# Sums of weights and low parts of keys and queries on GpSimd instead of VectorE

## The reference

```python
p_packed = sm_attn(p, k, v)              # 8 batches, 8 heads, 576 keys, head size 64
x = sm_attn(q, p_packed, p_packed)
h = x @ w_in                             # 512 -> 2048
y = (max(h, 0) + alpha * min(h, 0)) @ w_out
g = y @ w_gate                           # 512 -> 1536
out = (g * sigmoid(g) * (y @ w_val)) @ w_down
```

## Time and profile before

| | |
|---|---|
| three runs, us | 1558.52, 1558.85, 1555.52; median 1558.52 |
| profiled execution, us | 1558.1 |
| its span (first to last instruction), us | 1556.3 |
| TensorE busy, us | 1548.7 |
| VectorE busy, us | 1110.5 |
| ScalarE busy, us | 708.1 |
| GpSimd busy, us | 176.7 |
| granted clock of TensorE over the span | 1.000 |

### The profile page before, as it was taken

The page is one execution under the profiler, slowest core; times in us unless marked ns, Lnnn a source line. Parts: engine busy times, 40 slices in busy tenths (PEclk is TensorE's granted clock), DMA queues, the critical chain, the costliest instruction groups (busy, mean ns, idle before and its releaser), DMA issues.

```text
span 1556.3 us, 24850 instructions
## 1 busy us (share of the span) xinstructions
PE 1548.7 (100%) x9328; PEld 1435.6 (92%) x9328; DVE 1110.5 (71%) x1956; ACT 708.1 (45%) x1427; POOL 176.7 (11%) x194
## 2 busy tenths in 40 slices
PE   9999999999999999999999999999999999999999
PEld 6999999999999999999988888888888889999999
DVE  5565669877988779888755686557765685677666
ACT  4565567555765567655522252124422251234223
POOL 2654341000000010023200000000000000000000
PEclk9999999999999999999999999999999999999999
DMA  7443323442544345358466666676676668877866
GB/s 269 131 131 120 91 85 113 137 129 87 166 130 136 113 165 169 102 198 296 161 238 226 217 210 194 228 255 204 176 243 224 216 203 261 306 266 247 285 232 195
DMA packets 134503, 294.07 MB, mean 189 GB/s; under 512 B 13472, under 2 KB 44208, under 8 KB 134384
## 3 DMA queue, kind: packets, MB, share of 16 engines
q1 hardware_dynamic: 122400, 249.74, 49.7%
q0 software_dynamic: 11840, 42.48, 7.1%
q10 hardware_dynamic: 144, 0.26, 0.0%
HBM read 240.53 MB, written 51.90 MB: 188 GB/s over the span
## 4 chain that ended last, share of the span: by engine, by line
PE 96%; DVE 3%; DMA 1%; ACT 0%; issue 0%; DVEq 0%; ACTq 0%
PE acc L1070 14%; PE h L846 10%; PE h L848 10%; PE h L847 10%; PE side L846 9%; PE side L847 9%; PE side L848 9%; PE acc L1074 7%; PE acc L846 5%; PE acc L848 5%; PE acc L847 5%; DVE mixed L1536 1%; PE side L1004 1%; DVE piece L1536 1%; PE side L941 0%; DMA wring<-d_scratch 0%
## 5 line engine op out<-in xcount | busy, mean ns | idle before, releaser
L1070 PE MATMUL acc<-g,w 128*128 128x288 f32 x1792 | 272.8, 294 | 0.0
L1070 PEld LDWEIGHTS acc<-g,w 128*128 128x128 f32 x1792 | 248.9, 188 | 0.0
L1419 ACT ACTIVATE rows_b<-side 128x512 f32<-128x512 f32 (+1 forms) x60 | 33.4, 556 | 285.6 <-PE side L848 285.6
L1211 ACT ACTIVATE g<-floats 128x288 fp32r<-128x288 f32 x192 | 85.4, 445 | 165.0 <-DVE floats L1760 118.3
L1074 PE MATMUL acc<-g,w 128*128 128x288 f32 x896 | 156.2, 296 | 0.0
L846 PE MATMUL h<-attn,mixed 128*128 128x288 f32 x512 | 155.4, 303 | 0.5 <-DVE g L1536 0.5
L848 PE MATMUL h<-attn,mixed 128*128 128x288 f32 x512 | 151.1, 295 | 0.0
L847 PE MATMUL h<-attn,mixed 128*128 128x288 f32 x512 | 151.0, 295 | 0.0
L1074 PEld LDWEIGHTS acc<-g,w 128*128 128x128 f32 x896 | 131.2, 188 | 0.0
L1211 ACT ACTIVATE piece<-floats 128x512 fp32r<-128x512 f32 (+2 forms) x217 | 128.5, 616 | 3.2 <-PE side L848 2.9
L1536 DVE TENSOR_TENSOR g<-floats,g 128x288 fp32r<-128x288 f32 x192 | 87.3, 455 | 48.3 <-ACT g L1211 47.0
(11 more groups left out here) (324 smaller groups left out, 3934.8 us busy)
## 6 DMA issues: line engine op xcount, KB each, us to landing
ring<-w_scratch SPq DMA_DIRECT2D x90, 512.0 KB, 4.4
wring<-d_scratch SPq DMA_DIRECT2D x157, 256.0 KB, 2.9
ring_c<-w_scratch SPq DMA_DIRECT2D x60, 512.0 KB, 4.1
w_scratch<-piece POOLq DMA_DIRECT2D x36, 512.0 KB, 3.9
floats<-w_in SPq DMA_DIRECT2D x64, 256.0 KB, 3.1
ring_b<-w_scratch SPq DMA_DIRECT2D x30, 512.0 KB, 4.9
ring<-d_scratch SPq DMA_DIRECT2D x46, 256.0 KB, 2.9
d_scratch<-piece POOLq DMA_DIRECT2D x42, 256.0 KB, 3.5
```

The source lines that it names most:

```text
L1070: pe.matmul(acc[:, m, 0:CH], w2[:, j, x, m * P:(m + 1) * P], g[:, s % 2, 0, :], start=False, stop=False)
L1211: return nc.scalar.activation(dst, src, ACT.Copy, **kw)
```

## The change

It does three things. The four sums of each of the 18 sets are made by GpSimd instead of VectorE, in the same four operations and at the same place of the plan. The low parts of all k and q pieces are GpSimd's, so 36 pieces behind slot 63 (q of batch 3, k and q of batches 4 to 7) move; v, w, g and s pieces behind slot 63 stay with VectorE. And since sums and low parts are now on two engines, two waits change: SP, before it loads over the raw buffer of a gate tile, waits for that set's sums as well as for its low part; and the sums wait for all transposes of the first softmax before them in the plan (`turned`), as they write over its buffer, and no longer for those of the batches whose `packedT` is past. `firsts_before` goes.

```diff
 POOL_SLOTS = 64
-BY_POOL = [p for p in PIECES if p[0] in "kvqwo" and PLACE["split", p] < PLACE["y", POOL_SLOTS - 1]]
+BY_POOL = [p for p in PIECES if p[0] in "kq" or p[0] in "vwo" and PLACE["split", p] < PLACE["y", POOL_SLOTS - 1]]
...
             def load(p):
                 if RAW_NO[p] >= RING:
-                    once.wait_ge(*low_of(RAWS[RAW_NO[p] - RING]))
+                    last = RAWS[RAW_NO[p] - RING]
+                    once.wait_ge(*low_of(last))
+                    if last[0] == "g":
+                        once.wait_ge(sums_step, 4 * last[1] + 4)
...
+            def sums(e):
+
+                _, j, half = e
+                g_no, v_no = ("g", j, 0), ("g", j, 1)
...
+                if half == 0:
+                    if j in STAGED:
+                        once.wait_ge(y_stored, 16 * before(e, "ycopy"))
+                    else:
+                        once.wait_ge(turned, before(e, "turn"))
+                    if j >= EARLY_KEEPS:
+                        once.wait_ge(packed_done, B - 1)
+                    if j:
+                        once.wait_ge(*low_of(("s", j - 1, 1)))
+                    for p in (g_no, v_no):
+                        once.wait_ge(raw_landed[raw_slot(p)], landed(p))
+                    nc.gpsimd.tensor_tensor(s1_, a21, a22, ALU.add).then_inc(sums_step, 1)
+                    nc.gpsimd.tensor_tensor(s3_, a11, a21, ALU.subtract).then_inc(sums_step, 1)
+                    return
+                once.wait_ge(sums_step, 4 * j + 1)
+                nc.gpsimd.tensor_tensor(s2_, s1_, a11, ALU.subtract).then_inc(sums_step, 1)
+                once.wait_ge(sums_step, 4 * j + 3)
+                nc.gpsimd.tensor_tensor(s4_, a12, s2_, ALU.subtract).then_inc(sums_step, 1)
...
             for e in PLAN:
                 if e[0] == "split" and e[1] in BY_POOL:
                     input_low(e[1])
+                elif e[0] == "sums":
+                    sums(e)
...
-            def sums(e):
...
-                        once.wait_ge(turned, ST * firsts_before(e))
...
-                    nc.vector.tensor_tensor(s1_, a21, a22, ALU.add).then_inc(sums_step, 1)
-                    nc.vector.tensor_tensor(s3_, a11, a21, ALU.subtract).then_inc(sums_step, 1)
...
-                elif e[0] == "sums":
-                    sums(e)
```

More of the change, by code:

```diff
@@ L612, in unsplit @@
             return weight_sums(p[1])[:, 512 * p[2]:512 * p[2] + 512] if p[0] == "s" else raw(p)
-        def firsts_before(e):
-            return before(e, "packedT")
         def y_block(name, k, h):
@@ L806, in input_low @@
                                         ).then_inc(input_split, 1)
+            def sums(e):
+                _, j, half = e
+                g_no, v_no = ("g", j, 0), ("g", j, 1)
+                a11, a22 = raw(g_no)[:, 0:256], raw(v_no)[:, 256:512]
+                a12, a21 = raw(g_no)[:, 256:512], raw(v_no)[:, 0:256]
+                if j >= NT2:
+                    a12, a21 = a21, a12
+                s1_, s2_, s3_, s4_ = [weight_sums(j)[:, 256 * i:256 * i + 256] for i in range(4)]
+                if half == 0:
[16 more added lines that the diff above has]
+                nc.gpsimd.tensor_tensor(s4_, a12, s2_, ALU.subtract).then_inc(sums_step, 1)
             pool.dma_start(alphas, alpha).then_inc(alpha_landed, 16)
```

## The result

| | kernel before | changed kernel |
|---|---|---|
| median, us | 1557.12 | 1561.23 |
| lowest to highest, us | 1555.52 to 1558.85 | 1558.48 to 1563.72 |
| runs | 10 | 10 |
| span of the profiled execution, us | 1556.3 | 1559.4 |

The ratio is 1.0026, interval [1.0016, 1.0036]: 4.1 us slower, where I had forecast 0.7 us faster and no measurable change. The granted clock is 1.00 in both traces.

A forecast was written before the change was run, and what follows sets the result against it. TensorE was taken as the bound, busy 1548.7 of 1556.3 us, with VectorE seldom ending its waits. -1.6 + 0.9 = -0.7 us gave 1557.4 on the profiled execution's 1558.1, or 1557.8 as median; range 1555.4 to 1564.1 us.

The forecast's parts named there:

- (e): VectorE operations with two SBUF inputs blocked by GpSimd, at slots 84 to 86 and 64 slots later: +0.9 us.
- (a): 57 us of low parts and sums leave VectorE, relieving dense windows 400 to 440 and 600 to 640 us: -1.6 us.
- three quiet windows: Stretches from 240 us on outside the two dense windows, where TensorE was said to be never idle.
- (b): Work added to GpSimd: 36 pieces, 52.4 us, and 72 sums at 0.7 us, 50 us; it has room.
- (c): GpSimd's moved pieces and sums arrive in time; tightest piece has 3.19 us, 1.6 us left: hidden.
- (d): GpSimd's queue behind stores, and SP's extra wait before reloading a gate tile's raw buffer, cost nothing.
- a second kind of duration of the low part of g: Sign of a right forecast: some VectorE low parts of g last 0.8 to 1.4 us, which is the port.
- port rival: GpSimd takes the port ahead of needed low parts in eight stretches with k pairs: +5.6, 1564.1 us; chance 0.20.
- GpSimd late: A GpSimd piece or sum stands behind a waiting store, stalling TensorE at four tightest pieces: +4, 1562.5 us; chance 0.04.
- 0.39 us records instead of 0.47: Sign of a right forecast: TensorE's matmuls at the pieces in the dense windows shorten from 0.47 to 0.39 us.

The follow-up runs named there:

- e3: Changed kernel with each GpSimd sum waiting for the one ahead to finish, leaving a gap between any two; 1556.15 us, ratio 0.9991 to the kernel before.
- e7: Changed kernel with only one gap more, between the second and third sum, two sums staying back to back; 1557.91 us, ratio 1.0003 to the kernel before.
- e10: e3 with the low parts of the v pieces behind slot 63 moved to GpSimd as well; 1557.90 us, ratio 1.0001 to the kernel before.
- e4: Changed kernel with the float g left in PSUM up to slot 247; 1561.88 us, ratio 1.0029 to the kernel before.
- e2: Kernel before with only the k and q pieces moved to GpSimd, sums staying on VectorE; 1558.59 us, ratio 1.0007 to the kernel before.
- e1: Changed kernel with the k and q pieces back on VectorE, only the sums on GpSimd; 1561.71 us, ratio 1.0034 to the kernel before.
- e6: e3 with the k and q pieces back on VectorE, so only sums with gaps on GpSimd; 1557.82 us, ratio 1.0004 to the kernel before.
- e9: e8 with each sum also made in two halves of 128 columns with waits between; 1557.24 us, ratio 0.9999 to the kernel before.
- e8: e3 with each k and q piece behind slot 63 in two halves of 288 columns, a wait between; 1555.43 us, ratio 0.9991 to the kernel before.

## Why the prediction was wrong

**The step that failed** is (e), in its last sentence: "Elsewhere the low part of g comes 1 to 5 us early and a block of at most 1.4 us mostly vanishes in it." A block is not at most 1.4 us. I had taken the one GpSimd subtraction of the earlier trace rows for the unit of blocking. The four sums are three without a pause and one behind it, and VectorE is sure to get in only at the pause: the low part of g takes 2.16 us at slot 119, 3.23 at the longest. e3 and e7 show this, for they change nothing but the pauses. With it falls the value taken in (a): a block of 2.2 us at the sums of slots 119 and 183 is carried through a chain without slack, and -1.6 us became 2 x 0.80 = +1.6.

By the steps:

- *(a) removed, -1.6 us.* Right in kind, too large. Without the long holds (e3) the dense windows are 0.36 and 0.32 us shorter; with them 0.80 and 0.82 longer. I had costed the 57 us as leaving VectorE; 41 of them came back as waiting inside its instructions. I had also called TensorE never idle in the three quiet windows. In the kernel before, the h tile of slot 209 is 0.29 us late by its starts (665.02); in e3 it is not, and the stage from slot 192 on is 0.32 us shorter.
- *(b) added to GpSimd.* Right: 56 pieces of 576 columns, total 292 us against 280. A sum takes 0.73 to 0.74 us undisturbed, forecast 0.65 to 0.75; the means of 803 to 1116 ns are sums that VectorE held up in turn.
- *(c) in time, (d) waits and queues.* Right: no wait of TensorE on a GpSimd piece or sum shows, nor on the reload of a raw buffer. e10 shows what lies beyond.
- *(e) the port.* The mechanism was right, and what would show it also (a second kind of duration of the low part of g). The place was wrong: slots 84 to 86, where I had put 0.45 us, lie in the stage that stayed 168.87 us. The bad order did occur there. GpSimd's pieces held up a low part of g (1.69 us) and the normalisation (1.56 us for 0.75), and the next low part of g, kept out by a sum, ended at 300.35. TensorE wanted it at 300.60, so 0.25 us of the 0.54 were left, as VectorE no longer has 1.42 us of pieces to make in between. The same holds 64 slots later, and the 0.36 us of that stage lie elsewhere, at two h tiles of slots 169 and 171. The Trainium skill, "SBUF — State Buffer", section "Who interferes with whom", which I had weighed, speaks of one instruction keeping the port for its length; the row at 396.33 shows a VectorE instruction kept out for three of GpSimd's. It had waited since before the second and the third of them began, and this is so at 14 of 20 ends of a sum. The measurement goes further than the page. e4 confirms its condition, two inputs in SBUF, for this subtraction (450 ns against 604).
- *(e), size.* +0.9 us was forecast; the blocking cost 1.6 in the dense windows (and took their gain), 0.4 between them, 1.3 behind slot 192.

Of the rivals, the *port rival* was nearest (chance 0.20, 1564.1 us): slower by 4.1 us and for its reason, but it put the cost at eight pairs of k pieces. e2 shows those at +1.7 us by the table, 1.2 of it at slot 209 alone, and 1.0007 in time; the sums without a pause carry the rest (e3). Its condition, a block longer than slack plus what VectorE has saved, was the right test, and I applied it to the wrong instructions. *GpSimd late* didn't happen. The statement that the dense windows would show 0.39 us records instead of 0.47 was wrong, and this was the sign I had named. A row for the test was at hand: `sums` in the diff issues s1, s3 and s2 without a wait that can hold between them, and 3 x 0.7 us behind slot 118, ahead of a window in which VectorE has 38.96 of 40 us, needed only to be written down.

That the parts do not add up (e1 +4.8, e2 +1.7, both together +3.3) is in the main slots 85, 149 and 209, as shown at e6. What stays open: what decides whether VectorE gets in between two sums without a pause, and the single late tiles of e9 and e10. I hold the latter for places where the order of arrival at the port happens to be bad, but this is argued and not shown. GpSimd work of the same kind added without moving any wasn't tried.

## What to carry to other kernels

Before work with two inputs in SBUF goes to GpSimd, list the VectorE instructions with two inputs in SBUF that run beside it (here a `tensor_scalar` with one was held up too), and set the longest row of GpSimd operations without a pause, not the longest operation, against the slack of each. This is the worst case (VectorE got in earlier at 6 of 20 ends of a sum), but the slack has to cover it. A wait of GpSimd for its own operation before cost it about 0.1 us each here, and two of them a set were worth 0.35% of the whole. A wait that is already met makes no pause. VectorE's busy time doesn't tell the relief: look whether the durations of its instructions stayed what they were.

## What the runs showed that I had not expected

- A VectorE subtraction of 288 columns with both inputs in SBUF, ready 0.30 us after GpSimd began, was kept out through three sums of 0.74 us issued back to back, and ended 0.32 us after the third. A pause of 0.07 to 0.09 us lets it in (0.78 us in e3), at each of 21 places in e3. Without a pause it stayed out at 14 ends of a sum and got in at 6.
- It goes both ways: a GpSimd sum of 0.74 us took 1.07 when VectorE came first.
- GpSimd's subtraction undisturbed, on 128 partitions: about 460 ns for 128 columns (e9), 735 for 256, 802 for 288 (e8), 1290 for 512 and 1435 for 576. Halving doesn't halve: 2 x 802 = 1604 ns against 1435.
